# A linear-attention and two-MLP kernel: the last key and value block of a unit with 128 rows instead of 64

## The chip, the cores and the metric

The kernel runs on one core of a Trainium2 chip. The metric is the device time of one execution in microseconds (us); the median over several runs counts. The engines are named as in the profile: PE (TensorE, matmuls) with its weight loads PEld, DVE (VectorE), ACT (ScalarE), POOL (GpSimd), and SP (SyncE), whose queue issues all DMAs.

## What is computed

The reference is attention without a score matrix, and two MLPs behind it. Cut to what matters:

```python
batch, n_heads, seq, head_dim = (8, 8, 576, 64)

def _attn_ref(q, k, v):
    q_s = softmax(q, axis=-1)              # over the 64 channels of a head
    k_s = softmax(k, axis=2)               # over the 576 tokens
    kv = np.einsum('bhsd,bhse->bhde', k_s, v)
    return np.einsum('bhsd,bhde->bhse', q_s, kv)

# then, on 4608 tokens x 512:
h = relu(x @ w_in) ** 2;  x = h @ w_out                          # 512 -> 2048 -> 512
xn = x / rms(x) * rms_g;  out = silu(xn @ w_gate) * (xn @ w_val) @ w_out   # 512 -> 1536 -> 512
```

Both softmaxes are written out in the reference as an exponential of the value less its maximum, divided by the sum plus 1e-9.

## The kernel before

The work is cut into units of the attention: a unit is one batch's pair of heads (`u = unit(b, c)`, c from 0 to 3), so that two heads of 64 channels fill 128 columns. There are 32 units, four for each of the eight batches. The 576 tokens of a unit make four blocks of 128 (`FULL`) and one of 64 (`TAIL`), five in all (`SJ`).

For each unit PE does a few rounds, small groups of matmuls into one PSUM bank each:

- KM (L1744), a transpose of the keys' negated maxima, so that DVE can add them to the keys (L1389), and ACT can take the exponential in place (L1058). This covers all five blocks with 128 rows; the rows of the fifth that are not the last 64 tokens hold copies of other tokens' keys.
- KV (L1741), the changed line: for each of the five blocks j one fp32 matmul, exponentials of the keys (128 channels, as weights) by values (128 channels and a 129th column of ones, which gives the sum of the exponentials). The fifth block takes 64 rows (partitions) of both. The trace shows each fp32 matmul as two records.
- Q0 and Q1 (L1756), transposes of the normalised queries, and X0 and X1 (L1760), the queries by the block-diagonal factor that DVE makes of the KV round with its sum (L1376 to L1384).

Batch 0 has buffers of its own and runs alone at the head. The units of batch b (1 to 7) are spread by a table (`UNIT_BASE`, `UNIT_PE`, `UNIT_DVE` and so on) over the steps in which PE does the first matrix product of batch b - 1, one step being six matmuls of 288 columns (about 0.8 us). Batch 0's product is the plain one (L1788 to L1790). For the others seven block products (T1 to T4 and B11, B21, B22) stand for eight (L1767 to L1769), each as three fp32r matmuls of a high and a low part. Every engine's program runs the same steps in order and waits for semaphores; the order within an engine is fixed. At the change from one batch to the next, the hand-over, PE needs the next batch's operands `TAR`, which ACT (L1107) and DVE (L1412) split into high and low parts from `xa`, the attention's output, or from POOL's sums of its blocks (L885 to L899).

The two value buffers `vn[0]` and `vn[1]` are [128, 5, 129]. SP's `load_v` writes the 128 value columns of four full blocks and of the first 64 rows of the fifth (L628, L629). POOL writes the constants at the head, one after another, each adding one to the semaphore `const_done`; among them are the columns of ones (L857, L858) and, last, the zeros of `bd` (L859). DVE waits for the full count before its first write of the block-diagonal factor (L1381), PE before the first unit of batch 1 (L1737). POOL's first work of the attention is a subtraction (L873) behind DVE's maximum.

Behind the attention part (from about 446 us on) come the second product of the first MLP (L1853 to L1855), the gated MLP (L1767 to L1769 again, on other buffers) and its last product (L1937 to L1939). None of them is touched.

Of the kernel before, what the change touches and what calls it, by code (L numbers as in the profile page):

```python
# [12 lines left out]
P = 128  # L13
# [3 lines left out]
FULL, TAIL = S // P, S % P  # L17
# [272 lines left out]
def build(nc, q4_d, q1_d, kT_d, k5_d, v4_d, v1_d, w1_d, s1_d, w2_d, wB_d, gv_d, out):  # L290
# [4 lines left out]
    with ctx:  # L295
# [75 lines left out]
        kT, qn, vn, kt = [None] * 2, [None] * 2, [None] * 2, [None] * 2  # L371
# [89 lines left out]
        o11_done, o12_done, o21_done, o22_done = sem("o11_done"), sem("o12_done"), sem("o21_done"), sem("o22_done")  # L461
        out_st = [[sem(f"out{half}_st{i}") for i in range(O_SETS)] for half in range(2)]

        CONSTS, CONSTS_ALONE, CONSTS_Q = 11, 6, 2
        STAT_OPS = 2 * KC - 1

        def f(ap):
            return ap.bitcast(F32)
# [6 lines left out]
        def unit(b, c):  # L475
            return b * KC + c + 1

        def bufs(b, c):

            if b == 0:  # L480
                return Bufs(kT_al[:, c], qn_al[:, c], vn_al[:, c], ekS_al[:, c], qT_al[:, c], bd_al[:, c],
                            kmax_al[:, c], qmax_al[:, c])
            i = c % 2
            return Bufs(kT[i][:, :], qn[i][:, :, :, :], vn[i][:, :, :], kt[i][:, :, :], qT[:, :], bd[:, :], kmax[:, :],
                        qmax[:, :, :])

        def loads(b, c):

            if b == 0:
                return (kT_al_in[c], 16), (q_al_in[c], 32), (v_al_in[c], 32)  # L490
            n = (b - 1) * (KC // 2) + c // 2 + 1
            return (kT_in[c % 2], 16 * n), (q_in[c % 2], 32 * n), (v_in[c % 2], 32 * n)

        def round_bank(n):
            return ALONE_BANK[n % ALONE_BANKS] if n < N_ALONE else psR[(n - N_ALONE) % 2]

        def wait_taken(eng, n):

            act, count = taken_no(n)
            eng.wait_ge(taken_act if act else taken_dve, count)  # L500
# [7 lines left out]
        def wait_bank(eng, n):  # L508

            if n < N_ALONE:  # L510
                if n >= ALONE_BANKS:
                    wait_taken(eng, n - ALONE_BANKS)
            elif n < N_ALONE + 2:
                wait_alone(eng, round_bank(n))
            else:
                wait_taken(eng, n - 2)
# [86 lines left out]
        def _(sp):  # L603
# [105 lines left out]
            def store_a(q):  # L709

                k, m = QUADS[q]
                first, w = tokens_of(k)
                _, _, _, a1, a2 = buffers(q)
                sp.wait_ge(a1_done, q + 1)
                sp.dma_start(a_d[:, m, first:first + w], a1[:, 0:w]).then_inc(a1_st[q % 2], 16)
                sp.wait_ge(a2_done, q + 1)
                sp.dma_start(a_d[:, m, first + w:first + 2 * w], a2[:, 0:w]).then_inc(a2_st[q % 2], 16)
# [127 lines left out]
        def _(pool):  # L845
            done = 0
            for fill in (
                lambda: nc.gpsimd.memset(f(ones[:, :]), 1.0),
                lambda: nc.gpsimd.memset(qn_al[TAIL:P, :, FULL], 0.0),
                lambda: nc.gpsimd.affine_select(out=ident[:, :], in_=f(ones[:, :]), compare_op=ALU.is_equal, fill=0.0,  # L850
                                                base=0, pattern=[[-1, P]], channel_multiplier=1),
                lambda: nc.gpsimd.memset(ek_al[:, :, S:SJ * P], 0.0),
                lambda: nc.gpsimd.memset(vn_al[:, :, :, P:P + 1], 1.0),
                lambda: nc.gpsimd.memset(bd_al[:, :, :], 0.0),
                lambda: nc.gpsimd.memset(qn[0][TAIL:P, FULL], 0.0),
                lambda: nc.gpsimd.memset(qn[1][TAIL:P, FULL], 0.0),
                lambda: nc.gpsimd.memset(vn[0][:, :, P:P + 1], 1.0),  # L857
                lambda: nc.gpsimd.memset(vn[1][:, :, P:P + 1], 1.0),  # L858
                lambda: nc.gpsimd.memset(bd[:, :], 0.0),  # L859
            ):  # L860
                if done:
                    pool.wait_ge(const_done, done)
                fill().then_inc(const_done, 1)
                done += 1
# [183 lines left out]
        def _(act):  # L1048
# [110 lines left out]
            for _, what, i in ALONE_ACT:  # L1159
                task(what, 0, i)  # L1160
# [87 lines left out]
            def silu2(q):  # L1248

                w = width(q)  # L1250
                act.wait_ge(gate2_done, q + 1)
                if q >= 2:
                    act.wait_ge(a2_st[q % 2], 16 * (q // 2))
                _, gate2, _, _, a2 = buffers(q)
                nc.scalar.activation(a2[:, 0:w], gate2[:, 0:w], ACT.Silu).then_inc(silu2_done, 1)
# [466 lines left out]
        def _(pe):  # L1722
            def do_round(kind, b, c):

                u = unit(b, c)
                n = ROUND_NO[b, kind, c]
                ps = round_bank(n - 1)
                half = int(kind[1]) if kind[1] in "01" else 0
                wait_bank(pe, n - 1)
                m = bufs(b, c)  # L1730
                if kind == "KV":
                    if b == 0:
                        wait_taken(pe, ROUND_NO[b, "K1", c] - 1)
                    else:
                        pe.wait_ge(k_exp, u)
                    if (b, c) == (1, 0):
                        pe.wait_ge(const_done, CONSTS)  # L1737
                    pe.wait_ge(*loads(b, c)[2])
                    for j in range(SJ):
                        rows = slice(0, P if j < FULL else TAIL)  # L1740
                        last = nc.tensor.matmul(ps[:, 0:P + 1], m.ekS[rows, j, :], m.v[rows, j, :], start=j == 0, stop=j == SJ - 1)  # L1741
                elif kind == "KM":
                    pe.wait_ge(k_max, u)
                    last = nc.tensor.transpose(ps[:, 0:P], m.kmax.to_broadcast([P, P]), ident[:, :])  # L1744
                elif kind == "K0":
                    pe.wait_ge(k_exp, u)
                    for j in range(FULL):
                        last = nc.tensor.transpose(ps[:, j * P:(j + 1) * P], ek_al[:, c, j * P:(j + 1) * P], ident[:, :])
                elif kind == "K1":
                    last = nc.tensor.transpose(ps[:, 0:P], ek_al[:, c, FULL * P:SJ * P], ident[:, :])  # L1750
                elif kind[0] == "Q":
                    pe.wait_ge(q_norm, u)
                    blocks = range(0, Q_CUT) if half == 0 else range(Q_CUT, SJ)
                    for j in blocks:
                        o = (j - blocks[0]) * P
                        last = nc.tensor.transpose(ps[:, o:o + P], m.q[:, j].rearrange("p h d -> p (h d)"), ident[:, :])  # L1756
                else:
                    wait_taken(pe, ROUND_NO[b, "KV", c] - 1)
                    wait_taken(pe, ROUND_NO[b, "Q1" if half else "Q0", c] - 1)
                    last = nc.tensor.matmul(ps[:, 0:TA], m.bd, m.qT[:, half * TA:(half + 1) * TA], start=True, stop=True)  # L1760
                last.then_inc(rnd_ready, 1)
# [182 lines left out]
            for _, what, c in ALONE_PE:  # L1944
                if what == "plain":
                    for half in range(2):
                        plain(*PLAIN[c], half)
                else:
                    do_round(what, 0, c)
            for n in range(STEPS_PLAIN):  # L1950
                if n // 2:
                    plain(*PLAIN[n // 2], n % 2)
                for what, b, c in PE_AT.get(n, []):
                    do_round(what, b, c)
            for q in range(PA, NQA):
                for n, i in enumerate(ORDER):
                    if i not in range(7):
                        if q > PA:
                            product_a(q - 1, i[0])
                    else:  # L1960
                        product_a(q, i)
                    for what, b, c in PE_AT.get(start_of(1) + 7 * (q - PA) + n, []):
                        do_round(what, b, c)
# [74 lines left out]
```

## Time and profile before

| | us |
|---|---|
| median of 3 runs | 1695.15 (1694.55 to 1697.12) |
| the profiled execution | 1696.13 |
| its span, first to last instruction | 1694.4 |
| PE busy | 1664.2 (98%) |
| PE weight loads busy | 1514.6 (89%) |
| DVE busy | 1161.0 (69%) |
| ACT busy | 613.7 (36%) |
| POOL busy | 588.5 (35%) |
| DMA, mean | 136 GB/s |

The profile is of one execution. Its spans overlap on PE: matmuls are pipelined, the end of each is modelled, and the start of the next often lies before it. What a matmul costs is therefore read from one start to the next, or from the chain of work that ended last, in which each piece has only the time that it added. "Idle before" an instruction is time in which its engine did nothing, with what ended it behind the arrow.

### The profile page before, as it was taken

Reading aid. Unit: us, or ns where it says so; the run is one execution under the profiler, and the core shown is the slowest. Engines: PE = TensorE matmul, PEld = TensorE weight load, DVE = VectorE, ACT = ScalarE, POOL = GpSimd, SP = SyncE. Lnnn points to the kernel's source line nnn. Section 1 sums busy time; section 2 is a strip of 40 time slices with the busy share of each in tenths; the row PEclk is TensorE's granted clock in tenths of the full one; section 3 lists DMA queues with packets and bytes.
Section 4 is the critical chain, followed back from the end, with each engine's and each line's share of the span. In section 5 each row is a group of like instructions: output and inputs, shape, how many; then the busy total and the mean of one; then the engine's idle time right before and its main releaser. Section 6 shows DMA issues by size and latency. Waiting matters only on the chain.

```text
span 1694.4 us, 26373 instructions
## 1 busy us (share of the span) xinstructions
PE 1664.2 (98%) x9926; PEld 1514.6 (89%) x9926; DVE 1161.0 (69%) x1747; ACT 613.7 (36%) x1050; POOL 588.5 (35%) x468
## 2 busy tenths in 40 slices
PE   7999999999999999999999999999999998999999
PEld 6999999999988888888888988988998987999998
DVE  6677676757576778888785665546555558878775
ACT  5543333333232323333324433323333334443432
POOL 3554323323102224342256745546455543000000
PEclk9999999999999999999999999999999999999999
DMA  7675446545373354344432222242321344444441
GB/s 256 203 232 172 151 149 198 167 154 163 113 244 92 119 174 124 113 124 124 125 112 100 106 87 97 97 137 82 107 90 65 109 134 138 146 140 149 146 141 52
DMA packets 150974, 230.06 MB, mean 136 GB/s; under 512 B 11840, under 2 KB 74304, under 8 KB 150848
## 3 DMA queue, kind: packets, MB, share of 16 engines
q1 hardware_dynamic: 150848, 228.38, 41.1%
q8 instruction: 80, 1.31, 0.3%
q14 instruction: 46, 0.38, 0.1%
HBM read 143.39 MB, written 84.93 MB: 135 GB/s over the span
## 4 chain that ended last, share of the span: by engine, by line
PE 88%; DVE 5%; POOL 3%; issue 2%; DMA 1%; ACT 1%; SPq 0%; POOLq 0%; ACTq 0%; DVEq 0%
PE bank L1767 15%; PE bank L1768 14%; PE bank L1769 14%; PE bank L1853 7%; PE bank L1855 7%; PE bank L1854 7%; PE bank L1937 5%; PE bank L1939 5%; PE bank L1938 5%; PE bank L1741 3%; PE bank L1760 2%; DVE TAR L1412 1%; PE bank L1756 1%; DMA h_scratch<-hb 1%; PE bank L1788 1%
## 5 line engine op out<-in xcount | busy, mean ns | idle before, releaser
L1767 PE MATMUL bank<-TR,SW 128*128 128x512 f32 (+1 forms) x840 | 308.8, 368 | 4.3 <-DVE group L1573 2.3
L1769 PE MATMUL bank<-TR,SW 128*128 128x512 f32 (+1 forms) x840 | 308.7, 368 | 0.0
L1768 PE MATMUL bank<-TR,SW 128*128 128x512 f32 (+1 forms) x840 | 308.6, 367 | 0.0
L1767 PE MATMUL bank<-TAR,SA 128*128 128x288 f32 x784 | 251.0, 320 | 5.5 <-DVE TAR L1412 2.8
L1768 PE MATMUL bank<-TAR,SA 128*128 128x288 f32 x784 | 231.1, 295 | 0.0
L1769 PE MATMUL bank<-TAR,SA 128*128 128x288 f32 x784 | 230.4, 294 | 0.0
L1853 PE MATMUL bank<-GH,W 128*128 128x512 f32 x576 | 224.3, 389 | 2.0 <-DVE GH L1432 2.0
L1855 PE MATMUL bank<-GH,W 128*128 128x512 f32 x576 | 224.2, 389 | 0.0
L1854 PE MATMUL bank<-GH,W 128*128 128x512 f32 x576 | 224.2, 389 | 0.0
L1937 PE MATMUL bank<-SW,OA 128*128 128x256 f32 x630 | 178.9, 284 | 3.2 <-DVE SW L1599 3.2
L1767 PEld LDWEIGHTS bank<-TR,SW 128*128 128x128 f32 x840 | 157.7, 188 | 25.1 <-DVE group L1573 2.7
L1123 ACT ACTIVATE GH<-g 128x512 fp32r<-128x512 f32 x144 | 91.2, 634 | 244.6 <-DVE g L1427 159.6
L1939 PE MATMUL bank<-SW,OA 128*128 128x256 f32 x630 | 178.9, 284 | 0.0
L1938 PE MATMUL bank<-SW,OA 128*128 128x256 f32 x630 | 178.8, 284 | 0.0
L1768 PEld LDWEIGHTS bank<-TR,SW 128*128 128x128 f32 x840 | 157.6, 188 | 19.9
L1769 PEld LDWEIGHTS bank<-TR,SW 128*128 128x128 f32 x840 | 157.6, 188 | 19.8
L1432 DVE TENSOR_TENSOR GH<-g,GH 128x512 fp32r<-128x512 f32 x144 | 138.8, 964 | 40.6 <-ACT GH L1123 40.5
L1767 PEld LDWEIGHTS bank<-TAR,SA 128*128 128x128 f32 x784 | 147.1, 188 | 12.9 <-DVE TAR L1412 4.2
L1768 PEld LDWEIGHTS bank<-TAR,SA 128*128 128x128 f32 x784 | 147.6, 188 | 2.6
L1769 PEld LDWEIGHTS bank<-TAR,SA 128*128 128x128 f32 x784 | 147.3, 188 | 0.0
L1004 POOL TENSOR_TENSOR group<-group,group 128x512 f32<-128x512 f32 (+1 forms) x60 | 70.9, 1182 | 201.9 <-DVE group L1573 201.5
L1853 PEld LDWEIGHTS bank<-GH,W 128*128 128x128 f32 x576 | 108.1, 188 | 25.1 <-DVE GH L1432 2.7
(172 smaller groups left out, 3346.0 us busy)
## 6 DMA issues: line engine op xcount, KB each, us to landing
h_scratch<-hb SPq DMA_DIRECT2D x128, 288.0 KB, 2.7
hst<-h_scratch SPq DMA_DIRECT2D x144, 256.0 KB, 2.7
araw<-a_scratch SPq DMA_DIRECT2D x18, 1536.0 KB, 6.8
a_scratch<-group SPq DMA_DIRECT2D x72, 256.0 KB, 2.0
xst<-xn_scratch SPq DMA_DIRECT2D x10, 1024.0 KB, 5.1
xn_scratch<-x SPq DMA_DIRECT2D x9, 1024.0 KB, 5.4
a_scratch<-group SPq DMA_DIRECT2D x48, 192.0 KB, 1.8
out<-ost SPq DMA_DIRECT2D x36, 256.0 KB, 2.0
```

The source lines that it names most:

```text
L1004: nc.gpsimd.tensor_tensor(a1, a1, val1, ALU.mult).then_inc(a1_done, 1)
L1123: nc.scalar.activation(GH[:, r % GH_RING, 0], g[:, r % G_RING], ACT.Copy).then_inc(ghi_done, 1)
L1432: nc.vector.tensor_tensor(GH[:, r % GH_RING, 1], g[:, r % G_RING], f(GH[:, r % GH_RING, 0]), ALU.subtract)\
L1767: nc.tensor.matmul(ps[:, 0:w], w_hi[:, cc], x_hi[:, c], start=opens and c == 0, stop=False, skip_group_check=True)
L1768: nc.tensor.matmul(ps[:, 0:w], w_lo[:, cc], x_hi[:, c], start=False, stop=False, skip_group_check=True)
L1769: last = nc.tensor.matmul(ps[:, 0:w], w_hi[:, cc], x_lo[:, c], start=False, stop=c == 1, skip_group_check=True)
L1853: nc.tensor.matmul(acc[c][:, :], W2[:, j, 0, cc], GH[:, r % GH_RING, 0], start=j == 0, stop=False, skip_group_check=True)
L1854: nc.tensor.matmul(acc[c][:, :], W2[:, j, 1, cc], GH[:, r % GH_RING, 0], start=False, stop=False, skip_group_check=True)
L1855: last = nc.tensor.matmul(acc[c][:, :], W2[:, j, 0, cc], GH[:, r % GH_RING, 1], start=False, stop=j == CA - 1, skip_group_check=True)
L1937: nc.tensor.matmul(ps, a_hi, w_hi, start=start, stop=False, skip_group_check=True)
L1938: nc.tensor.matmul(ps, a_lo, w_hi, start=False, stop=False, skip_group_check=True)
L1939: last = nc.tensor.matmul(ps, a_hi, w_lo, start=False, stop=stop, skip_group_check=True)
```

## The change

In batches 1 to 7 the fifth block of the KV round is taken with 128 rows, as the other four are. The 64 rows of the values that hold no token, with their part of the column of ones, are set to zero once at the head by two more memsets on POOL, placed behind those that write the ones; so the exponentials of the copied keys in these rows add nothing. The count of constants goes from 11 to 13. Batch 0 keeps its 64 rows.

```diff
-        CONSTS, CONSTS_ALONE, CONSTS_Q = 11, 6, 2
+        CONSTS, CONSTS_ALONE, CONSTS_Q = 13, 6, 2
@@ POOL's constants
                 lambda: nc.gpsimd.memset(vn[0][:, :, P:P + 1], 1.0),
                 lambda: nc.gpsimd.memset(vn[1][:, :, P:P + 1], 1.0),
+                lambda: nc.gpsimd.memset(vn[0][TAIL:P, FULL], 0.0),
+                lambda: nc.gpsimd.memset(vn[1][TAIL:P, FULL], 0.0),
                 lambda: nc.gpsimd.memset(bd[:, :], 0.0),
@@ PE, the KV round
                     for j in range(SJ):
-                        rows = slice(0, P if j < FULL else TAIL)
+                        rows = slice(0, P if j < FULL or b else TAIL)
                         last = nc.tensor.matmul(ps[:, 0:P + 1], m.ekS[rows, j, :], m.v[rows, j, :], start=j == 0, stop=j == SJ - 1)
```

## Rows read from the trace of the kernel before

**Rows 1.** The page's first part: busy us, share of the span, instructions.

```profile
PE 1664.2 (98%) x9926; PEld 1514.6 (89%) x9926; DVE 1161.0 (69%) x1747; ACT 613.7 (36%) x1050; POOL 588.5 (35%) x468
```

**Rows 2.** Busy us by stretch: PE, PEld, DVE, ACT, POOL; clock, DMA share, GB/s.

```profile
42.00:98.00 56.00, 55.62 (x403) 53.53 (x403) 40.19 (x68) 27.80 (x50) 29.15 (x28) 1.00 0.67 213
98.00:156.00 58.00, 57.01 (x415) 54.87 (x413) 43.94 (x89) 25.68 (x52) 32.52 (x31) 1.00 0.60 195
```

**Rows 3.** PE waits, 98 to 445 us (total, times, longest); timeline, two hand-overs.

```profile
PE bank L1767 <- DVE TAR L1412: 2.4, 5, 0.5
...
156.63 0.40 PE L1767 MATMUL bank<-TAR,SA 128*128 128x288 f32 x1 [0.48 <-DVE TAR L1412]
...
214.67 0.40 PE L1767 MATMUL bank<-TAR,SA 128*128 128x288 f32 x1 [0.49 <-DVE TAR L1412]
```

**Rows 4.** PE's groups by shape, line 1741 (rows*columns of the array first).

```profile
L1741 PE MATMUL bank<-vn,kt 128*128 128x129 f32 x224 | 30.2, 277 | 1.0 <-ACT qT L1077 1.0
L1741 PE MATMUL bank<-vn,kt 64*128 64x129 f32 x56 | 13.6, 323 | 0.0
...
L1741 PEld LDWEIGHTS bank<-vn,kt 128*128 128x128 f32 x224 | 27.7, 191 | 1.8 <-ACT qT L1077 1.2
L1741 PEld LDWEIGHTS bank<-vn,kt 64*128 64x128 f32 x56 | 8.3, 185 | 3.4
```

**Rows 5.** Timeline (start, us), one unit, cut at 54.02, 54.80, 55.00, 55.20 us.

```profile
53.83 0.38 PE L1741 MATMUL bank<-vn,kt 128*128 128x129 f32 x2
...
53.83 1.06 PE L1741 MATMUL bank<-vn,kt 128*128 128x129 f32 x8
...
53.83 1.36 PE L1741 MATMUL bank<-vn,kt 128*128 128x129 f32 x9
...
53.83 1.47 PE L1741 MATMUL bank<-vn,kt 128*128 128x129 f32 x10
```

**Rows 6.** The chain in order of time (start, us): KV round, L1756, L1760.

```profile
54.00 1.31 PE bank L1741 x10
55.31 0.33 PE bank L1788
55.64 0.13 PE bank L1789
...
135.47 0.33 PE bank L1756 x3
135.80 0.14 PE bank L1767
...
142.31 0.48 PE bank L1760 x2
142.79 0.13 PE bank L1767
```

**Rows 7.** POOL's timeline at the head of the program.

```profile
3.16 0.20 POOL L855 MEMSET qn<- 64x128 f32 x1
...
4.01 0.20 POOL L859 MEMSET bd<- 128x128 f32 x1
6.24 1.26 POOL L873 TENSOR_TENSOR qn_alone<-qn_alone,qmax_alone 128x640 f32<-128x640 f32 x1 [2.03 <-DVE qmax_alone L1352]
```

**Rows 8.** The chain at the hand-overs: 88 to 90 us, 147 to 157 us.

```profile
88.87 0.15 PE bank L1790
...
147.12 0.15 PE bank L1769
147.66 0.75 DVE TAR L1412
...
154.97 1.62 DVE TAR L1412
```

**Rows 9.** All engines' waits, 98 to 445 us, the longest (as rows 3).

```profile
POOL qn L873 <- DVE qmax L1352: 84.5, 22, 5.3
```

**Rows 10.** The table by stretch, at the lower clock.

```profile
1422.00:1426.00 4.00, 4.00 (x23) 4.00 (x22) 3.97 (x5) 1.85 (x3) 0.69 (x1) 0.57 0.18 69
```

## The prediction

> **What bounds the kernel now.** I read first the page's busy shares: TensorE (PE) is busy for 98% of the span, VectorE (DVE) for 69%, and nothing else for more than 36% apart from the weight loads, which run beside the matmuls [rows 1]. That is an average, so I looked next at the stretches in which the changed line runs. The table by stretch cuts the attention part at the hand-overs from batch to batch. PE is busy for 55.62 of the 56 us from 42 us on, and for 57.01 of the next 58 us [rows 2]. One batch takes 58.04 us: PE starts the first matmul behind the same wait at 156.63 us and at 214.67 us [rows 3]. So in this stage a nanosecond taken from PE's own stream is worth a nanosecond, unless it only makes a wait longer. How that can happen is the third thing to read: PE's waits. From 98 us to 445 us the longest entry is DVE's split of the next batch's operand at the hand-overs, five times, 2.4 us in all [rows 3].
>
> **What the change takes away.** Line 1741 multiplies the exponentials of the keys with the values, five blocks of tokens for each unit (a batch's pair of heads). Each of these fp32 matmuls leaves two records, so a unit has ten: eight with 128 rows of the array, and two with 64 rows for the last block. In batches 1 to 7 there are 28 units, hence the 224 and 56 records [rows 4].
>
> What one 64-row block costs can't be read from the mean durations, since the ends of matmuls are modelled and overlap. I read the starts. The timeline of the unit at 53.83 us, cut at later and later points, shows the group grow: two records end after 0.38 us, eight after 1.06 us, so one more 128-row record adds (1.06 - 0.38) / 6 = 0.113 us. The ninth, which is the first with 64 rows, adds 0.30 us (1.06 to 1.36) and the tenth 0.11 us (to 1.47) [rows 5]. The chain of waits shows the other side of the block: the first matmul of the product behind it has 0.33 us on the chain, and the next one 0.13 us [rows 6].
>
> Two things could be charged for the 0.30 and the 0.33: the change of the number of rows, once down to 64 and once up to 128, or simply the change from one kind of work to another. The nearest rows tell them apart. Behind the transposes of the queries (L1756), which also end a group and have another shape than the products, but use all 128 rows, the first matmul of the product has 0.14 us on the chain, and behind the two matmuls of L1760, 128 rows again, 0.13 us [rows 6]. So it is the rows. What I see is that the weight load of the 64-row matmul starts only when the matmuls before it are nearly through, and that of the next 128-row matmul likewise, where otherwise a load starts one matmul ahead.
>
> With 128 rows in all five blocks the ten records should run at one pace: 1.06 + 2 x 0.113 = 1.29 us instead of 1.47, which is 0.18 us less, and the matmul behind has 0.13 instead of 0.33, which is 0.20 us less. That is 0.38 us a unit, and 28 x 0.384 = 10.8 us.
>
> The bounds of this term. A pass over 64 more rows could cost something of its own: the rows of the same line bound it, because the eight 128-row records already run at 0.113 us with all 128 rows, and that is the pace I have used. The least that the rows allow is the difference of the mean durations, 56 x (323 - 277) ns = 2.6 us [rows 4]; it leaves out the follower and trusts modelled ends, so it serves only as a lower end. The most is that the follower would take its 0.13 us and both 64-row records theirs at the fastest step of a 128-row record, 0.11 us, which gives 0.39 us a unit, 10.9 us. I take 10.8, for the chain and the cut timeline agree on it.
>
> On this the Trainium skill has two rules that lead apart. TensorEngine Tiling (Array Packing), section Key Properties, says that changing the tiling mode, not only the tile, drains the engine; here the matmul after the change of rows is indeed late by about 0.2 us each way, and by that rule the sum would be the one above. TensorE: Matmul & The Clock Gate, on loading the stationary operand, says that the time goes by columns and that the row count does not matter; for the bare load the rows agree (185 ns against 191 ns [rows 4]), and by that rule alone the change would bring nothing, which is the first rival below.
>
> **What the change adds.** Two memsets on GpSimd (POOL) at the head, each 64 partitions x 129 values. The row of nearly the same size (64 x 128, L855) has 0.20 us; with a wait between, POOL's queue grows by some 0.5 us. It now ends with the memset of bd at 4.01 us and POOL's next work starts at 6.24 us after 2.03 us idle, waiting for DVE's maximum [rows 7]. The 0.5 us lies in that idle time: cost 0. Without that cover, it would be 0.5 us at most, once. The constants' count of 13 is waited for by DVE before its first write of the block-diagonal factor and by PE before the first unit of batch 1. Nothing else than these instructions' own successors is queued behind them, and both come after POOL's row at 6.24 us, where the count is long complete: cost 0. The DMAs are as before, for the values' load still writes only the 64 rows of real tokens. ACT's exponential already covers all 128 rows of the fifth block before the change, so no engine but PE has another instruction in the loop.
>
> **What is late next.** The saving is made in the rounds that stand at, for instance, 101.7, 113.7, 125.6 and 137.5 us of a batch. It counts only if the wait at the hand-over doesn't grow by as much. The chain there: PE is let go at 156.63 us by a DVE split [rows 3], and DVE has been on the chain since 147.27 us, where the piece before it is a PE matmul of the product line (L1769) [rows 8]. The four rounds lie before that release. So the whole stretch of DVE work moves up with PE, the wait of 0.48 us stays, and the batch goes from 58.04 to 58.04 - 4 x 0.384 = 56.5 us. The hand-over at 96 to 101 us has the same form: DVE, ACT and POOL work that goes back to a PE matmul at 88.87 us [rows 8], so the four units of batch 1, which run in the stage before, count as well. Between 98 and 445 us DVE, ACT and POOL wait for one another and for PE, the longest in total for DVE; a DMA is not in the list [rows 9]. So no transfer can come late from a shift of 1.5 us in 58. Behind 445 us everything is as before, only earlier.
>
> **The rivals.**
> 1. The two slow steps belong to something else than the number of rows (the end of a long accumulation, or reading the values' tile), or more rows bring back what the switch costs. For it: the two 64-row records are always the last of the group, so the position is never seen apart from the rows. Against: the rows behind L1756 and L1760. Time: 1695.15 us, no change.
> 2. The saving is made, but the hand-overs eat a part: if DVE's run of work were late for another reason than PE, PE's wait at each of the six hand-overs at which it waits for DVE (97 to 388 us) would grow by up to 1.54 us. Half of the saving of the 24 units before them lost is 6 x 0.77 = 4.6 us, which gives 1689.0 us; all of it lost 9.2 us, 1693.6 us. Against: the release at 147.27 us by PE [rows 8].
> 3. Slower: in the run of DVE work before each hand-over one split has 1.62 us where the first has 0.75 us [rows 8]; POOL works at the same time. If the earlier rounds slid three more DVE steps of that run under POOL's work, each would cost some 0.87 us more: 6 x 2.6 = 15.7 us against 10.8 us won, 1700.1 us. It decides from a growth of over 1.8 us a hand-over (10.8 / 6) on. Against: DVE's, POOL's and PE's work there is all released from the same PE stream, so their places to one another stay.
> 4. That the change does not do what it says can hardly be: the extra rows of the values and of their column of ones are zero, and 128 rows are written into the instruction.
>
> **How the numbers follow.** The profiled execution took 1696.13 us, of which 1694.4 us are its span and 1.7 us lie around it; with 10.8 us less it would have 1685.3 us. The median of the runs is 1695.15 us, 1.0 us below the profiled one, and the prediction is for such a median: 1695.15 - 10.8 = 1684.4 us. Chances: the full saving, within a microsecond or two, 0.82; rival 2, 0.09 (half of it still ends faster by over 0.2%); rival 1, 0.06; rival 3, 0.03. What a measurement of this kernel can tell from no change is about 0.2%, 3.4 us: the three runs before span 1694.55 to 1697.12. The low end of the range is the full saving with the 0.6 us by which the median stands over its lowest run, and another microsecond for the half-speed stretch below; the high end takes in the smaller third of rival 2. Range 1682.8 to 1688.2 us. Faster by over 0.2%: 0.82 + 0.08 = 0.90; within: 0.06 + 0.01 = 0.07; slower: 0.03.
>
> **What would show it.** The line's records should all have 128 rows, 280 of them, near 0.113 us from start to start. The matmul behind each group should have 0.13 us on the chain. A batch should take 56.5 us between two hand-overs, with the wait for DVE still 0.48 us. POOL's first subtraction should stay near 6.24 us. Behind the attention part the trace should be the same, shifted. What would make it wrong: hand-over waits that grow, or a different count of stretches at the lower clock. There is one now, from 1422 us on: for 4 us the granted clock averages 0.57 [rows 10], between its two levels of 2.4 and 1.2 GHz. It costs some 4 x 0.43 = 1.7 us and may come or go; I expect it to stay, for nothing near it is touched.

## The result and the profile after

The changed kernel takes 1685.12 us in the median of six runs (1684.85 to 1685.76), the kernel before, run beside it, 1695.75 us (1694.55 to 1698.53). The ratio is 0.9936 with a 95% interval of 0.9926 to 0.9946: faster by 0.64%, 10.6 us. The forecast was 1684.4 us, between 1682.8 and 1688.2 us, from a saving of 10.8 us. The profiled executions took 1696.13 and 1685.14 us, 11.0 us apart.

The line's groups by shape, which answer to [rows 4] (the line is 1743 now):

```profile
L1743 PE MATMUL bank<-vn,kt 128*128 128x129 f32 x280 | 36.5, 277 | 1.0 <-ACT qT L1079 1.0
L1743 PEld LDWEIGHTS bank<-vn,kt 128*128 128x128 f32 x280 | 34.0, 191 | 1.8 <-ACT qT L1079 1.2
```

All 280 records have 128 rows. The timeline of the same unit as in [rows 5], cut behind the eighth record and behind the group (start, us):

```profile
54.10 1.05 PE L1743 MATMUL bank<-vn,kt 128*128 128x129 f32 x8
...
54.10 1.28 PE L1743 MATMUL bank<-vn,kt 128*128 128x129 f32 x10
```

The last two records add 0.23 us, where they added 0.41 us; 1.29 us for the ten was forecast. The chain in order of time shows the matmul behind the group, which answers to [rows 6]:

```profile
54.26 1.12 PE bank L1743 x10
55.38 0.13 PE bank L1790
```

It has 0.13 us now instead of 0.33, and the group 1.12 instead of 1.31. Two rows carry the result through the attention part. The answer for the line in the kernel before and in the changed one has the shortest, middle and longest record in ns, and then the starts of the first and the last record:

```profile
L1741 PE MATMUL bank<-vn,kt x280: 271/275/378, 41.1 to 428.7; 128*128 128x129 f32 x112, 64*128 64x129 f32 x28
```

```profile
L1743 PE MATMUL bank<-vn,kt x280: 271/275/378, 41.8 to 419.0; 128*128 128x129 f32 x140
```

From the first to the last record it was 387.6 us and is 377.2 us, 10.4 us less. Between these two starts lie the slow steps inside 28 groups and behind 27 of them, 55 in all. Two of them gave nothing, as is shown below; the other 53 gave 10.4 / 53 = 0.196 us each. The hand-overs, as in [rows 3] (timeline; wait in brackets), and PE's waits from 98 to 434 us:

```profile
154.61 0.40 PE L1769 MATMUL bank<-TAR,SA 128*128 128x288 f32 x1 [0.49 <-DVE TAR L1414]
...
211.07 0.40 PE L1769 MATMUL bank<-TAR,SA 128*128 128x288 f32 x1 [0.49 <-DVE TAR L1414]
...
PE bank L1769 <- DVE TAR L1414: 2.6, 6, 0.5
```

A batch takes 56.46 us instead of 58.04, and PE waits 0.49 us at each of these hand-overs, where it waited 0.48 or 0.49. The sixth wait in the list is new. It stands behind the first KV round of batch 2, in the hand-over that begins at 96 us. The timeline there, from this KV round to the next round (X, the queries by the block-diagonal factor), before and after:

```profile
101.68 1.58 PE L1741 MATMUL bank<-vn,kt 128*128 128x129 f32 x10 [0.99 <-ACT qT L1077]
...
106.49 0.65 PE L1760 MATMUL bank<-qT,bd 128*128 128x288 f32 x2
```

```profile
100.78 1.39 PE L1743 MATMUL bank<-vn,kt 128*128 128x129 f32 x10 [0.99 <-ACT qT L1079]
...
104.71 0.40 PE L1769 MATMUL bank<-TAR,SA 128*128 128x288 f32 x1 [0.16 <-DVE TAR L1414]
...
105.61 0.65 PE L1762 MATMUL bank<-qT,bd 128*128 128x288 f32 x2
```

The two rounds are 4.81 us apart before and 4.83 us after. The KV round is shorter, but PE then comes to the product before DVE's split is there, and the unit as a whole saves nothing. So 27 of the 28 units count.

### The profile page after: what moved, and what is told of

Same layout as the page of the kernel before. It is cut to its first block, busy times and chain, and to the rows that moved or that the text cites. A ratio compares the mean times of both kernels' runs of the same rounds, so it can differ in the third digit from the quotient of the medians.

```text
span 1683.4 us, 26375 instructions
## 1 busy us (share of the span) xinstructions
PE 1654.7 (98%) x9926; PEld 1511.5 (90%) x9926; DVE 1160.1 (69%) x1747; ACT 613.5 (36%) x1050; POOL 589.4 (35%) x470
## 3 DMA queue, kind: packets, MB, share of 16 engines
q8 instruction: 80, 1.31, 0.3%
## 4 chain that ended last, share of the span: by engine, by line
PE 88%; DVE 5%; POOL 3%; issue 1%; DMA 1%; ACT 1%; SPq 0%; POOLq 0%; DVEq 0%; ACTq 0%
PE bank L1769 14%; PE bank L1771 14%; PE bank L1770 14%; PE bank L1855 7%; PE bank L1857 7%; PE bank L1856 7%; PE bank L1939 5%; PE bank L1940 5%; PE bank L1941 5%; PE bank L1743 2%; PE bank L1762 2%; DVE TAR L1414 1%; PE bank L1758 1%; DMA h_scratch<-hb 1%; PE bank L1790 1%
```

## The experiments

The theory: PE loses about 0.195 us at each change between 128 and 64 rows, up or down, and nothing in this kernel hides it. The rivals: the slow steps belong to the end of the group; each matmul with few rows is dear by itself; the hand-overs take up a part. The kernel before, run beside them, had a median of 1696.14 us for the first four kernels and of 1696.06 us for the last four.

**The 64-row block first instead of last.**

```diff
-                    for j in range(SJ):
+                    order = (4, 0, 1, 2, 3) if b else (0, 1, 2, 3, 4)
+                    for j in order:
...
-start=j == 0, stop=j == SJ - 1)
+start=j == order[0], stop=j == order[-1])
```

> The kernel before, with the 64-row block taken first in each KV round of batches 1 to 7 instead of last. The sum over blocks is the same. Theory (PE loses about 0.195 us at each change between 128 and 64 rows, wherever it stands): there are still two changes a unit, so the time is that of before within 0.2%; the first of the ten records starts late, and so does the one behind the second, while the product matmul behind the group has 0.13 us on the chain. Rival (the slow steps belong to the end of the accumulation, not to the rows): the slow steps stay at the ninth and tenth record and at the product behind them.

Measured: ratio to before 0.9994 (0.9984 to 1.0003). The timeline of one unit of it, cut behind the second, the third and the fourth record, and then the chain behind the group:

```profile
54.34 0.49 PE L1742 MATMUL bank<-vn,kt 64*128 64x129 f32 x2
...
54.34 0.79 PE L1742 MATMUL bank<-vn,kt 64*128 64x129 f32 x3
...
54.34 0.91 PE L1742 MATMUL bank<-vn,kt 64*128 64x129 f32 x4
...
54.41 1.51 PE bank L1742 x10
55.91 0.13 PE bank L1789
```

The slow step has moved with the block: the third record, the first with 128 rows (the row names the shape of the first of its group), adds 0.30 us, the fourth 0.12 us, and the product behind the group has 0.13 us. The group takes 1.51 us on the chain, 0.39 more than with 128 rows throughout, so both slow steps are in it now. Group and follower have 1.64 us together, as in [rows 6]. The position is out as a cause.

**Two 64-row blocks, apart and side by side.** These two belong together: the same number of 64-row matmuls, but four changes of the row count in a unit in the one, and two in the other.

```diff
-                        rows = slice(0, P if j < FULL else TAIL)
+                        rows = slice(0, P if j < FULL and not (b and j == 1) else TAIL)    # two_apart
+                        rows = slice(0, P if j < FULL and not (b and j == 3) else TAIL)    # two_adjacent
```

> The kernel before, with 64 rows also in the second of the five blocks (64 tokens of each unit of batches 1 to 7 are left out of the sum), so that four changes of the row count stand in a unit instead of two. Theory: 28 x 2 x 0.195 = 10.9 us slower than before. Rival (a 64-row matmul is cheap where it doesn't end the accumulation): as before. Rival (hand-overs take up what PE gains or loses): well under 10.9 us.

> The kernel before, with 64 rows also in the fourth block, next to the fifth (64 tokens of each unit of batches 1 to 7 are left out). Still two changes of the row count in a unit, but twice the 64-row matmuls. Theory (the price is for the change, not for the matmul with few rows): within 0.2% of before. Rival (each 64-row matmul costs 0.39 us more than one with 128 rows): 28 x 0.39 = 10.9 us slower, as with the two apart.

Measured: apart 1.0065 (1.005 to 1.008), 1706.92 us, 10.8 us more than before; side by side 0.9995 (0.9986 to 1.0005). The chain through one unit, first of the kernel with the two apart:

```profile
54.04 1.70 PE bank L1741 x10
55.74 0.33 PE bank L1788
```

and with the two side by side:

```profile
52.91 1.31 PE bank L1741 x10
54.22 0.33 PE bank L1788
```

Apart, the group takes 0.39 us more; side by side it takes what it takes in the kernel before, though it has twice as many records of 64 rows. So the price is for the change and not for the matmul with few rows. It also bears on the hand-overs: they pass on a loss of 0.39 us a unit in full. The line's starts in the kernel with the two apart:

```profile
L1741 PE MATMUL bank<-vn,kt x280: 271/275/378, 40.8 to 439.2; 128*128 128x129 f32 x84, 64*128 64x129 f32 x56
```

They span 398.4 us, 10.8 more than before, 0.39 us for each of the 28 groups. Taking the 28 pairs away saved 10.4 us between the same two starts, 0.39 us for each unit that counts.

**The memsets alone.**

```diff
-                        rows = slice(0, P if j < FULL or b else TAIL)
+                        rows = slice(0, P if j < FULL else TAIL)
```

> The changed kernel with its two memsets and its count of 13, but with 64 rows in the KV round again: one part alone. Theory: within 0.2% of before, POOL's first subtraction near 6.2 us. Rival (the head's queue counts): 0.5 us slower.

Measured: 0.9999 (0.999 to 1.0008). POOL's timeline at the head of it:

```profile
4.03 0.20 POOL L859 MEMSET vn<- 64x129 f32 x1
4.29 0.20 POOL L860 MEMSET vn<- 64x129 f32 x1
4.54 0.21 POOL L861 MEMSET bd<- 128x128 f32 x1
6.13 1.26 POOL L875 TENSOR_TENSOR qn_alone<-qn_alone,qmax_alone 128x640 f32<-128x640 f32 x1 [1.38 <-DVE qmax_alone L1354]
```

The last constant is 0.5 us later than in [rows 7], and the idle time before the subtraction is shorter by about as much. The saving is all of the other part.

**96 rows, and 32 rows.** What counts as a change: any other number than 128?

```diff
-                        rows = slice(0, P if j < FULL or b else TAIL)
+                        rows = slice(0, P if j < FULL else 96 if b else TAIL)      # rows96, from the changed kernel
+                        rows = slice(0, P if j < FULL else 32 if b else TAIL)      # rows32, from the kernel before
```

> The changed kernel with rows 0 to 95 in the last block of batches 1 to 7 instead of all 128 (the 32 rows of zeros beyond the tokens are of no use; the result is that of the reference). Theory (the price is for a change of the array's mode, 64 rows or the whole, and 96 rows run in the mode of 128): as the changed kernel, 0.64% faster than before. Rival (any other number of rows than 128 costs the two changes): as before. Which it is was not shown by any row.

> The kernel before with 32 rows in the last block of batches 1 to 7 (32 tokens of each unit are left out). Theory (a price for the change, whatever the smaller number): within 0.2% of before. Rival (the price grows or falls with the number of rows, for instance because the load or the pass takes time by rows): off by some us, with another step at the ninth and tenth record.

Measured: 96 rows 0.9934 (0.992 to 0.9947), 32 rows 0.9998 (0.9989 to 1.0007). The groups by shape of the one, and then the chain through one of its units:

```profile
L1743 PE MATMUL bank<-vn,kt 96*128 96x129 f32 x56 | 10.8, 274 | 0.0
L1743 PEld LDWEIGHTS bank<-vn,kt 96*128 96x128 f32 x56 | 8.4, 190 | 0.0
...
54.22 1.12 PE bank L1743 x10
55.34 0.13 PE bank L1790
```

and the same of the other:

```profile
L1741 PE MATMUL bank<-vn,kt 32*128 32x129 f32 x56 | 13.6, 321 | 0.0
L1741 PEld LDWEIGHTS bank<-vn,kt 32*128 32x128 f32 x56 | 8.2, 183 | 3.4
...
53.06 1.31 PE bank L1741 x10
54.37 0.33 PE bank L1788
```

With 96 rows there is nothing of a change, and with 32 rows it costs what it costs with 64. So in these runs 96 rows go with the whole array. The price doesn't follow the number of rows, it is paid or not. The loads show it too: ahead of the loads of the short block the load side of PE is idle for 3.4 us in all with 32 rows, as with 64 [rows 4], and for nothing with 96. Whether the late load causes the slow step, or both come from one thing, no run here separates.

**Half of the units.**

```diff
-                        rows = slice(0, P if j < FULL or b else TAIL)
+                        rows = slice(0, P if j < FULL or b and c < 2 else TAIL)
```

> The changed kernel with 128 rows only in the first two units of each batch from 1 to 7 (14 of 28), 64 rows in the two others. Theory (a nanosecond is worth a nanosecond, the hand-overs keep their waits): half the saving, 5.4 us, 1690 us against a median near 1695.5. Rival (the hand-over chain forgives a part, so that the first units or the last count for more): clearly more or less than 5.4 us.

Measured: 0.9965 (0.9952 to 0.9979), median 1690.93 us, 5.1 us less than the kernel before. The starts:

```profile
L1743 PE MATMUL bank<-vn,kt x280: 271/275/378, 40.6 to 423.0; 128*128 128x129 f32 x126, 64*128 64x129 f32 x14
```

They span 382.4 us, 5.2 less than before. The times alone allow a saving of 3.6 to 8.1 us; the starts are what makes it sharp. The first unit of batch 2 is among the 14 and has the new wait here as well (0.15 us), so 13 of them count, at 0.39 us each 5.1 us. The saving goes by the number of units, but for that one.

**Batch 0 as well.** It is the only place left where the rows change.

```diff
-        CONSTS, CONSTS_ALONE, CONSTS_Q = 13, 6, 2
+        CONSTS, CONSTS_ALONE, CONSTS_Q = 14, 7, 2
...
+                lambda: nc.gpsimd.memset(vn_al[TAIL:P, :, FULL], 0.0),
...
-                    nc.scalar.activation(m.ekS[0:TAIL, FULL, :], ps[0:TAIL, 0:P], ACT.Copy).then_inc(taken_act, 1)
+                    nc.scalar.activation(m.ekS[:, FULL, :], ps[:, 0:P], ACT.Copy).then_inc(taken_act, 1)
...
-                        rows = slice(0, P if j < FULL or b else TAIL)
+                        rows = slice(0, P)
```

> The changed kernel with 128 rows in the four units of batch 0 as well (ACT copies all 128 rows of the transposed fifth block, and one more memset of 64 x 516 values on POOL sets the values' spare rows to zero ahead of the constants that PE waits for). Three of these units stand on the chain at the head in the trace, so the most is 4 x 0.39 = 1.6 us less than the changed kernel; the theory that PE is not the bound in this stage but waits for ACT and DVE in between gives 0 to 1 us less; the rival, that the longer queue of memsets (about 0.6 us) delays the first unit, gives up to 0.6 us more.

Measured: 0.9931 (0.9917 to 0.9945) of before, median 1685.40 us (1683.98 to 1686.16). The changed kernel has 0.9936 (0.9926 to 0.9946), measured in another session. Nothing that can be told apart is gained, as is to be expected of at most 1.6 us in a stage where PE waits for others. The change itself works in batch 0 too. The chain through the last unit of batch 0, first in the changed kernel, then in this one:

```profile
25.04 1.55 PE bank L1743 x10
26.59 1.17 PE bank L1762 x4
```

```profile
23.28 1.35 PE bank L1744 x10
24.64 0.97 PE bank L1763 x4
```

That is 0.20 us less in each of the two pieces. Whether it reaches the total stays open. The start of the first record of batch 1 lies at 39.7 us in this kernel, the lowest of all ten, but the others have it anywhere from 40.1 (two_adjacent) to 41.8 us, without any change to batch 0. And from the last long DVE piece on the chain (L1602, at 1406.86 us) to the end this execution took 276.1 us, the changed kernel's from the same piece 275.0 us, with 25 steps at the lower clock's pace instead of 15.

## Why the prediction was right

- **Two slow steps and two changes.** The term was 0.384 us a unit; the chain through one unit shows 0.39 us (1.31 + 0.33 before, 1.12 + 0.13 after), and the stretch of all units 0.39 (2 x 0.196). The rows of the transposes and of L1760 had pointed to the rows and not to the kind of work, and the block moved to the front showed it. What the prediction couldn't tell from the trace of before, the position of the block, is what tail_first settled; the choice between the matmul and the change is settled by the pair two_apart and two_adjacent.
- **More rows cost nothing by themselves.** The added 64 rows run at the pace of the others, 0.23 us for two records. Rival 1 falls.
- **PE's stream is the bound in this stage, and the hand-overs move with it.** Measured at 56.46 us a batch, against 56.5. Rival 2 falls, but for one unit, by the waits after (0.49 us each, as before) and by half_units; rival 3 by the same rows. That is the unit at 100.8 us: the sum took all 28 units at full value, and this one brought nothing. With 27 units it would have been 10.4 us, and the forecast 0.4 us higher. The prediction looked only at whether the old waits would grow, and not for a place where PE, being earlier, would meet a wait that was not there.
- **The memsets cost nothing**, shown alone.
- **What is behind it moves as a whole**, right in the sum and not in detail. Of the 11.0 us between the two profiled executions the rounds from the first to the last record give 10.4 and the follower of the last one 0.2. The rest is a head 0.7 us longer and the stretch behind. There, PE's waits at the change to the second product are these, before and after:

```profile
PE bank L1767 <- ACT hb L1148: 2.7, 2, 1.6
PE bank L1853 <- DVE GH L1432: 1.5, 1, 1.5
```

```profile
PE bank L1769 <- ACT hb L1150: 1.8, 2, 1.4
PE bank L1855 <- DVE GH L1434: 1.4, 1, 1.4
```

They are 1.0 us shorter. The chain in that stretch goes through a store of the first product, 8.75 and 7.55 us from issue to landing before, 7.53 and 7.73 us after. In the kernel with 96 rows the same two waits sum to 4.3 us, although its PE stream in the attention part is that of the changed kernel; one store there took 9.08 us, and from 464 us on the granted clock averaged 0.57 for 4 us. So this differs from execution to execution, and I count it neither for the change nor against it. That the two executions came out 11.0 us apart, so near to 10.8, is then partly luck: the head (0.7 us longer) and these waits (1.0 us shorter) happened to offset each other and the unit that brought nothing.

- **The stretch at the lower clock** was expected to stay. It stayed, and two more came:

```profile
18.00:22.00 4.00, 4.00 (x17) 3.49 (x18) 3.83 (x9) 1.50 (x4) 2.60 (x2) 0.57 1.04 367
...
1390.00:1394.00 4.00, 4.00 (x12) 3.15 (x11) 2.77 (x4) 1.36 (x3) 4.00 (x5) 0.57 0.35 131
1410.50:1414.50 4.00, 3.79 (x19) 3.82 (x20) 4.00 (x5) 1.85 (x3) 1.20 (x1) 0.57 0.21 80
```

In the table by stretch the clock is the number before the last two. The stretch at 18 us lies in the head; tail_first and the kernel with 96 rows have a head as long as the changed kernel's without one, so it isn't shown to cost anything. The stretch at 1411 us is the one of [rows 10]. The one at 1390 us holds matmuls of the gated MLP back, but it stands ahead of a wait for DVE at the end of that stage, which took it up. PE's waits there, 1395 to 1425 us before and 1384 to 1414 us after:

```profile
PE bank L1767 <- DVE group L1573: 2.3, 1, 2.3
PE bank L1767 <- DVE group L1590: 1.8, 1, 1.8
```

```profile
PE bank L1769 <- DVE group L1575: 2.2, 1, 2.2
```

The wait of 1.8 us for L1590 is gone. The chain there goes through POOL and DVE and not through these matmuls.

The prediction priced the stretch of [rows 10] at 1.7 us and left a microsecond for it in the range. That term was too large. The steps at the lower clock and then at the full clock, in the chain of the kernel before:

```profile
1423.49 0.21 PE bank L1939
...
1425.83 0.12 PE bank L1939
```

Fifteen steps are longer by 0.09 us, 1.4 us in all. But tail_first and two_adjacent have no such stretch behind 1404 us, and from the start of the same DVE piece on the chain (L1599, 1419.40 us in the kernel before) to the end of the span they take 274.8 and 274.7 us, against 275.0 us before and after the change. Without the stretch PE comes to another wait, here in two_adjacent:

```profile
PE bank L1937 <- DVE OA L1605: 0.5, 1, 0.5
```

So the stretch costs 0.2 to 0.3 us of the total. Where a wait follows, it costs less than its steps say.

The upper end of the range, 1688.2 us, is not quite what its words give: a third of rival 2's 9.2 us on top of 1684.4 is 1687.5 us. Nothing hangs on it here.

## What to carry to other kernels

When an fp32 matmul of 64 or 32 rows stands alone among matmuls of the whole array, fill it up to the whole (with zeros in one operand and finite numbers in the other), or put all short ones side by side, if PE is the bound there. What counts is the number of changes and not of short matmuls, and the price is seen in the steps from start to start and in the matmul behind the group, hardly in the mean duration: that alone would have given 2.6 of the 10.8 us. Before counting such a saving in full, follow the chain at the next wait of the engine back to what released it, and look for operands that now arrive just in time: an earlier engine can meet a new wait there.

## What the runs showed of the hardware

- A change between 64 or 32 rows and 128 rows costs about 0.2 us each way on fp32 matmuls of 129 columns at full clock (1.64 us for group and follower against 1.25 us, two changes), and the same for 64 and 32 rows. Other types, other widths and a change between 64 and 32 rows were not tried.
- 96 rows don't count as a change: 0.9934 against 0.9936 for all 128. Of numbers between 64 and 96 nothing was tried.
- The Trainium skill (TensorEngine Tiling (Array Packing), section Key Properties) states that a change of the tiling mode drains the engine. The runs agree in that each change costs; the drain itself is not seen in them. The same page of the Trainium skill, section Available Configurations, names row tilings of 128, 64 and 32 rows. The runs agree: 96 rows, for which there is none, go with 128.
- The Trainium skill (TensorE: Matmul & The Clock Gate, section Step-by-step: what each phase is for) states that the number of rows doesn't matter for the time of a load. The bare load agrees: 183 ns with 32 rows, 185 with 64, 190 with 96 and 191 with 128. The step from start to start is about 0.2 us longer all the same where the number of rows changes to or from 64 or 32.
